# A second raw tile, loads in another order, statistics one tile per period, and another cut of the last odd fold in a three-stage kernel

## What is computed

```python
def phi(x):
    proj = einsum('bhsd,df->bhsf', x, w_phi)            # 64 -> 128
    proj = proj - max(abs(proj), axis=-1, keepdims=True)
    return concatenate([exp(proj), exp(-proj)], axis=-1)
q_p, k_p = phi(q), phi(k)
kv, z = einsum('bhsf,bhsd->bhfd', k_p, v), sum(k_p, axis=2)
x = einsum('bhsf,bhfd->bhsd', q_p, kv) / (einsum('bhsf,bhf->bhs', q_p, z) + 1e-6)
u = x + real(fft(fft(x, axis=1), axis=2))               # heads joined to 512 columns
y = u + relu(layernorm(u) @ w1a) @ w2a                  # w1: 512 x 2048, w2: 2048 x 512
out = y + relu((layernorm(y) * g) @ w1b) @ w2b
```

## Time and profile before

| | us |
|---|---|
| median of 3 runs (lowest to highest) | 1062.37 (1058.77 to 1062.54) |
| the profiled execution | 1061.2 |
| its span | 1059.1 |
| PE busy | 1043.5 |
| DVE busy | 668.2 |
| ACT busy | 527.9 |
| POOL busy | 382.2 |

### The profile page before, as it was taken

The page is one execution under the profiler, slowest core; times in us unless marked ns, Lnnn a source line. Parts: engine busy times, 40 slices in busy tenths (PEclk is TensorE's granted clock), DMA queues, the critical chain, the costliest instruction groups (busy, mean ns, idle before and its releaser), DMA issues.

```text
span 1059.1 us, 17436 instructions
## 1 busy us (share of the span) xinstructions
PE 1043.5 (99%) x6294; PEld 964.1 (91%) x6294; DVE 668.2 (63%) x1155; ACT 527.9 (50%) x958; POOL 382.2 (36%) x365
## 2 busy tenths in 40 slices
PE   8999999999899999999999999999999999999998
PEld 8999999999889899899898899889899899999897
DVE  5675776798775557754586564864568554674443
ACT  5756565676544436344354445444454444544341
POOL 4413333254343426242451433523444323532210
PEclk9999999999999999999999999999999999999999
DMA  5242121210123121222122122222114221142201
GB/s 140 69 108 68 35 69 35 67 46 13 56 65 119 50 72 60 75 65 81 42 79 78 43 80 60 64 77 69 52 61 139 61 80 60 60 135 77 61 7 60
DMA packets 68626, 72.47 MB, mean 68 GB/s; under 512 B 24256, under 2 KB 49088, under 8 KB 68544
## 3 DMA queue, kind: packets, MB, share of 16 engines
q1 hardware_dynamic: 68384, 71.30, 22.6%
q10 hardware_dynamic: 160, 0.07, 0.0%
HBM read 66.10 MB, written 4.72 MB: 67 GB/s over the span
## 4 chain that ended last, share of the span: by engine, by line
PE 88%; DVE 6%; issue 2%; ACT 2%; DMA 1%; SPq 1%; POOL 1%; DVEq 0%; ACTq 0%; POOLq 0%
PE bank L1102 34%; PE bank L1079 30%; PE bank L383 6%; PE bank L369 5%; PE bank L331 4%; PE bank L352 3%; PE bank L616 2%; PE bank L596 2%; PE bank L1038 2%; DVE stats L1384 2%; DMA rawqk<-qkT 1%; PE bank L325 1%; DVE hid L1358 1%; DVE w1op L1286 1%; DVE part_s L1328 0%
## 5 line engine op out<-in xcount | busy, mean ns | idle before, releaser
L1102 PE MATMUL bank<-w2op,hid 128*128 128x512 f32 x1728 | 426.1, 391 | 0.0
L1102 PEld LDWEIGHTS bank<-w2op,hid 128*128 128x128 f32 x1728 | 321.8, 188 | 56.6 <-issue 0.5
L1079 PE MATMUL bank<-x_T,w1op 128*128 128x384 f32 x1152 | 208.9, 336 | 0.0
L1079 PEld LDWEIGHTS bank<-x_T,w1op 128*128 128x128 f32 x1152 | 201.7, 188 | 3.8
L1250 POOL TENSOR_TENSOR w_sums<-st_w 128x256 f32<-128x256 f32 x48 | 44.8, 933 | 411.2 <-DVE w1op L1286 405.2
L1079 PE MATMUL bank<-x_B,w1op 128*128 128x384 f32 x864 | 176.2, 339 | 0.9 <-DVE part_s L1328 0.9
L1079 PEld LDWEIGHTS bank<-x_B,w1op 128*128 128x128 f32 x864 | 151.9, 188 | 10.0 <-issue 1.3
L1299 DVE TENSOR_TENSOR w2op<-st_w,w2op 128x1024 fp32r<-128x1024 f32 x48 | 65.8, 1372 | 98.7 <-ACT w2op L1295 98.7
L1358 DVE SCALAR_TENSOR_TENSOR hid<-part_s,hid 128x384 fp32r<-128x384 f32 x141 | 97.5, 718 | 37.3 <-ACT hid L1354 37.1
L1354 ACT ACTIVATE hid<-part_s 128x384 fp32r<-128x384 f32 x141 | 72.9, 524 | 28.6 <-DVE part_s L1328 28.3
L399 POOL TENSOR_TENSOR qk_lo<-rawqk,qk_hi 128x640 fp32r<-128x640 f32 x28 | 42.7, 1548 | 119.8 <-ACT qk_hi L393 119.8
(11 more groups left out here) (171 smaller groups left out, 1610.3 us busy)
## 6 DMA issues: line engine op xcount, KB each, us to landing
st_w<-w1a SPq DMA_DIRECT2D x24, 512.0 KB, 3.4
st_w<-w2a SPq DMA_DIRECT2D x24, 512.0 KB, 3.7
st_w<-w1b SPq DMA_DIRECT2D x24, 512.0 KB, 3.3
st_w<-w2b SPq DMA_DIRECT2D x24, 512.0 KB, 3.7
rawqk<-qkT SPq DMA_DIRECT2D x16, 288.0 KB, 3.8
rawqk<-qkT SPq DMA_DIRECT2D x16, 256.0 KB, 4.0
v<-v SPq DMA_DIRECT2D x16, 256.0 KB, 3.1
out<-xall SPq DMA_DIRECT2D x16, 256.0 KB, 2.1
```

Source lines behind the costliest of these rows:

```text
L1079: last = nc.tensor.matmul(dst, w1op[g % 2][:, a, W1OP.index(w), c, :], xop[x][:, b, c, :], start=name in ("M2", "M1", "M7") and k_ == 0, s ...
L1102: last = nc.tensor.matmul(acc[t0 + t][:, :], hid[name, g % 2][:, x, P * t:P * (t + 1)], w2op[g % 2][:, y, j, :], start=first and k_ == 0, ...
```

## The change

Pair 1 gets a raw tile of its own (`rawqk_second`), with its own zeroing by POOL and loading semaphore; the other pairs keep the shared tile. The two halves of w_phi are loaded first, one by SP and one by ACT; q of pair 0 comes by SP and k by ACT, with a semaphore each, and pair 1's load follows at once. The values of pair 0, pair 2's load and the constants come behind that. PE does 23 instead of 26 transposes of the identity first, the 26 in the middle go, and in slot 1 the first three units of pair 1 run before the transposes of round 0 and the 22 transposes of the identity. POOL makes the low part of pair 1. ACT and POOL split all constants in slot 2.

The two W1 loads of slot 4 are issued in slots 4 and 6. The root of the first block moves inside slot 13. The statistics get a second set of tiles, and those of block i + 2 are made one tile per period in periods 2 to 7 of block i; those of block 1 stand in the last batch's part (four tiles) and behind it (two). The root of the next block moves to period 0, the reciprocal to the head of period 1.

For the last fold the odd part no longer waits for the extra row, and the extra row waits for the odd part. POOL's even fold no longer waits for DVE's odd fold, but its next two low parts wait for the low parts of W1's second block. The orders of ACT, DVE and PE in that part change.

```diff
@@ -104,14 +104,14 @@
-    stats, o = at("stats", [P, BT, 6], F32, o)
-    mv, o = at("mv", [P, BT, 2], F32, o)
+    stats, o = at("stats", [P, 2, BT, 6], F32, o)
+    mv, o = at("mv", [P, 2, BT, 2], F32, o)
+    rstd, o = at("rstd", [P, 2, BT], F32, o)
...
-    rstd, o = at("rstd", [P, BT], F32, o)
-    wphi, o = at("wphi", [P, FEAT], F32, o)
...
-    pad, o = at("pad", [P, 1], F32, o)
...
+    wphi, o = at("wphi", [P, FEAT], F32, KEEP)
+    raw_second, o = at("rawqk_second", [P, 2, QW], F32, o)
@@ -238,10 +238,11 @@
-    s_qk, s_v, s_zero, s_w0 = sem("qk_loaded"), sem("v_loaded"), sem("zeros_ready"), sem("w_phi_split")
+    s_qk, s_v, s_zero, s_w0 = [sem("qk_even_loaded"), sem("qk_odd_loaded")], sem("v_loaded"), sem("zeros_ready"), sem("w_phi_split")
...
+    s_first, s_zero2, s_w0_lo = [sem("first_q_loaded"), sem("first_k_loaded")], sem("second_zeros_ready"), sem("w_phi_lo")
@@ -385,19 +386,27 @@
+    def raw_qk(g):
+        return raw_second if g == 1 else rawqk
+    def act_first_hi(act, w):
+        act.wait_ge(s_first[w], 48)
+        nc.scalar.copy(sqk["hi"][0][:, w, :], rawqk[:, w, :]).then_inc(qk_hi, 1)
...
-        act.wait_ge(s_qk, 48 * (g + 1))
+        act.wait_ge(s_qk[g % 2], 48 * ((g + 1) // 2))
...
-            nc.scalar.copy(sqk["hi"][g % 2][:, w, :], rawqk[:, w, :]).then_inc(qk_hi, 1)
-    def split_lo(eng, unit, g):
-        for w in range(2):
+            nc.scalar.copy(sqk["hi"][g % 2][:, w, :], raw_qk(g)[:, w, :]).then_inc(qk_hi, 1)
+    def split_lo(eng, unit, g, parts=(0, 1)):
+        for w in parts:
...
-            unit.tensor_tensor(sqk["lo"][g % 2][:, w, :], rawqk[:, w, :], f32(sqk["hi"][g % 2][:, w, :]), ALU.subtract)\
-                .then_inc(qk_lo, 1)
+            unit.tensor_tensor(sqk["lo"][g % 2][:, w, :], raw_qk(g)[:, w, :], f32(sqk["hi"][g % 2][:, w, :]),
+                               ALU.subtract).then_inc(qk_lo, 1)
@@ -498,15 +507,25 @@
+    QK_PARTS = ((slice(D, P), slice(0, MT * P), slice(0, MT * P)),
+                (slice(0, D), slice(0, S), slice(0, S)),
+                (slice(D, P), slice(MT * P + TAIL, QW), slice(MT * P, S)))
+    def load_first(eng, w):
+        for k_, (rows, dst, cols) in enumerate(QK_PARTS):
+            if k_ == 1:
+                eng.wait_ge(s_zero, 1)
+            eng.dma_start(rawqk[rows, w, dst], qkT[0][rows, w, cols]).then_inc(s_first[w], 16)
...
-        need(sp, qk_lo, 2 * g)
-        need(sp, qk_hi, 2 * g)
-        if g == 0:
-            sp.wait_ge(s_zero, 1)
-        for rows, dst, cols in ((slice(0, D), slice(0, S), slice(0, S)),
-                                (slice(D, P), slice(0, MT * P), slice(0, MT * P)),
-                                (slice(D, P), slice(MT * P + TAIL, QW), slice(MT * P, S))):
-            sp.dma_start(rawqk[rows, :, dst], qkT[g][rows, :, cols]).then_inc(s_qk, 16)
+        if g == 1:
+            sp.wait_ge(s_zero2, 1)
+        else:
+            need(sp, qk_lo, 2 * g if g > 2 else 2)
+            need(sp, qk_hi, 2 * g if g > 2 else 2)
+        for rows, dst, cols in QK_PARTS:
+            sp.dma_start(raw_qk(g)[rows, :, dst], qkT[g][rows, :, cols]).then_inc(s_qk[g % 2], 16)
@@ -619,6 +638,8 @@
+        if (b, h) == (B - 1, 1):
+            act.wait_ge(o_done, 4 * B)
@@ -644,7 +665,8 @@
-        eng.wait_ge(s_exrow, 2 * (q_ + 1))
+        eng.wait_ge(fin, H * b + 4 * (h + 1))
+        eng.wait_ge(s_exrow, 2 * (q_ + (q_ < 2 * B - 1)))
@@ -802,7 +824,13 @@
         if l >= 0 and g > 1:
             pe_transpose(pe, l, 0)
         for u in range(3):
+            if g == 0 and u == 2:
+                pe.wait_ge(s_w0, 2)
+                pe.wait_ge(s_w0_lo, 2)
             pe_unit(pe, g, u)
+        if g == 1:
+            pe_transpose(pe, l, 0)
+            pe_warm_on(pe, bank[5], WARM - 4)
         if l < 0:
             pe_unit(pe, g, 3)
             pe_unit(pe, g, 4)
@@ -934,10 +962,15 @@
+        if g == 2:
+            act.wait_ge(s_raw, 16 * 5)
+            act_const_hi(act, "cs")
...
-            for n in ("cd", "sd", "alt"):
-                act_const_hi(act, n)
+            act_const_hi(act, "ss")
+            act_const_hi(act, "cd")
+        if g == STD_SLOT:
+            act_std(act, 0)
@@ -947,13 +980,15 @@
+        if g == 2:
+            act_const_hi(act, "sd")
...
+        if g == 2:
+            act_const_hi(act, "alt")
...
-        if g == STD_SLOT:
-            act_std(act, 0)
@@ -1119,9 +1154,9 @@
         pe_product(pe, 0, "M1")
         pe_stepA(pe, B - 1, "S1")
         pe_product(pe, 0, "M6")
+        pe_product(pe, 0, "M7")
         pe_stepA(pe, B - 1, "C1")
         pe_stepA(pe, B - 1, "CX")
-        pe_product(pe, 0, "M7")
         for name in B_OUT[:HT]:
             pe_stepB(pe, B - 1, name)
         pe_product(pe, 0, "M5")
@@ -1377,31 +1412,29 @@
-            if i == NB - 1:
+            if BT * i + tiles[-1] >= len(FULL):
...
-        need(dve, mv_done, BT * i)
+        need(dve, xn_done, BT * (i - 1))
...
-            nc.vector.bn_stats(stats[:, t, :], utile(i, t)).then_inc(st_done, 1)
-        need(dve, xn_done, BT * i)
-        need(dve, sd_done, i)
+            nc.vector.bn_stats(stats[:, i % 2, t, :], utile(i, t)).then_inc(st_done, 1)
...
-            nc.vector.bn_aggr(mv[:, t, :], stats[:, t, :]).then_inc(mv_done, 1)
+            nc.vector.bn_aggr(mv[:, i % 2, t, :], stats[:, i % 2, t, :]).then_inc(mv_done, 1)
...
-        nc.scalar.activation(std[:, :], mv[:, :, 1], ACT.Sqrt, bias=epsc[:, 0:1]).then_inc(sd_done, 1)
+        nc.scalar.activation(std[:, :], mv[:, i % 2, :, 1], ACT.Sqrt, bias=epsc[:, 0:1]).then_inc(sd_done, 1)
...
-        nc.vector.reciprocal(rstd[:, :], std[:, :]).then_inc(rs_done, 1)
+        nc.vector.reciprocal(rstd[:, i % 2, :], std[:, :]).then_inc(rs_done, 1)
...
-        nc.vector.tensor_scalar(xn[k % 2][:, :], utile(i, t), mv[:, t, 0:1], rstd[:, t:t + 1],
+        nc.vector.tensor_scalar(xn[k % 2][:, :], utile(i, t), mv[:, i % 2, t, 0:1], rstd[:, i % 2, t:t + 1],
@@ -1433,8 +1466,6 @@
-            if n == 1 and nxt:
-                act_std(act, i + 1)
@@ -1443,6 +1474,8 @@
+            if n == 0 and nxt:
+                act_std(act, i + 1)
@@ -1463,8 +1496,8 @@
-                dve_ln_stats(dve, i + 1, range(BT))
-            late = n == FP_ - 1 or n == 1
+                dve_ln_rstd(dve, i + 1)
+            late = n == FP_ - 1
@@ -1477,14 +1510,14 @@
-            if n == 1 and nxt:
-                dve_ln_rstd(dve, i + 1)
...
+            if n >= TR0 and i + 2 < 2 * NB:
+                dve_ln_stats(dve, i + 2, range(n - TR0, n - TR0 + 1))
@@ -1550,19 +1583,20 @@
-            sp_qk(sp, 0)
+            sp.dma_start(wphi[0:D, :], w_phi).then_inc(s_const, 16)
+            load_first(sp, 0)
+            sp_qk(sp, 1)
...
+            sp_qk(sp, 2)
...
-            sp_qk(sp, 1)
...
-                if g + 1 < PAIRS:
+                if 1 < g < PAIRS - 1:
...
-                if g == 4:
-                    sp_w1(sp, 0)
-                    sp_w1(sp, 1)
+                if g in (4, 6):
+                    sp_w1(sp, g // 2 - 2)
@@ -1583,6 +1617,7 @@
+            nc.gpsimd.memset(raw_second[:, :, MT * P:QW], 0.0).then_inc(s_zero2, 1)
@@ -1595,13 +1630,13 @@
+                if g == 0:
+                    pool.wait_ge(qk_lo, 2)
+                    split_lo(pool, nc.gpsimd, 1)
...
-                if g == 0:
-                    for n_, n in enumerate(("cs", "ss")):
+                if g == 2:
+                    for n_, n in enumerate(("cs", "ss", "cd", "sd")):
...
-                if g == 2:
-                    for n_, n in enumerate(("cd", "sd")):
-                        split_const(pool, nc.gpsimd, 2 + n_, n)
@@ -1614,8 +1649,8 @@
-            pool.wait_ge(oo_done, 2 * B)
...
+            pool.wait_ge(w1_lo, 6)
@@ -1626,25 +1661,24 @@
-            for half in range(2):
-                act.dma_start(wphi[D * half:D * (half + 1), :], w_phi).then_inc(s_const, 16)
+            act.dma_start(wphi[D:P, :], w_phi).then_inc(s_const, 16)
+            load_first(act, 1)
...
-                nc.scalar.copy(wbd["hi"][rows, FEAT * a:FEAT * (a + 1)], wphi[rows, :])
+                last = nc.scalar.copy(wbd["hi"][rows, FEAT * a:FEAT * (a + 1)], wphi[rows, :])
+            last.then_inc(s_w0, 1)
+            act_first_hi(act, 0)
...
-            act_split_qk(act, 0)
+            act_first_hi(act, 1)
+            act_split_qk(act, 1)
...
-            act_split_qk(act, 1)
+            act_q_copy_out(act, 0, 0)
...
-            act.wait_ge(s_raw, 16 * 5)
-            act_q_copy_out(act, 0, 0)
-            act_const_hi(act, "cs")
...
-            act_const_hi(act, "ss")
+            act_split_qk(act, 2)
...
-            act_split_qk(act, 2)
@@ -1665,23 +1699,23 @@
             act_x_hi(act, 0, 2)
             act_x_hi(act, 0, 3)
+            t_split(act, B - 1, "S0", True)
             act_exrow(act, B - 1, 1)
-            t_split(act, B - 1, "S0", True)
+            act_fold_hi(act, B - 1, 1, True)
             t_split(act, B - 1, "C0", True)
```

(36 more changed lines are left out.)

## The result

The median falls from 1060.57 us (four runs, 1058.19 to 1062.54) to 1049.95 us (four runs, 1049.78 to 1050.14): a ratio of 0.9903, with a 95% interval of 0.988 to 0.9927. The forecast was 1051.1. The profiled execution took 1050.14 us with a span of 1048.2, against 1061.2 and 1059.1 before.

The account below looks back on a forecast made before the run. PE, busy in 99% of the span, was taken as the bound, so savings had to come from its time line. Gains 2.3 + 1.8 + 0.5 + 1.7 + 1.8 + 2.0 = 10.1 us took 1061.2 to 1051.1 us, range 1046.5 to 1056.0.

Parts of the forecast that it names:

- A: The start: new PE order and earlier pair 1 load gain 1.8 us, earlier first projection 0.5; 2.3 us in all.
- rival (1): At the start, the first projection doesn't move: A is 1.8 us, total 1051.6 us; chance 0.15.
- B: W1 loads: one instead of two ahead of pair 6's load lets its cast start earlier; gain 1.8 us (1.3 to 1.9).
- C: Slot 13: root and its table load move two copies ahead, exponentials of q come earlier; gain 0.5 us (0.2 to 0.7).
- D: Last batch's fold: earlier Fourier steps, no half clock, but DVE late with two collisions; gain 1.7 us (0 to 4.4).
- E: First expert block: six statistics leave its second period and PE's waits behind them go; gain 1.8 us (0.9 to 2.2).
- F: Next four expert blocks: waits before the transposes go, 0.5 us each; gain 2.0 us (1.6 to 2.4).
- (5): Slower: with fewer warm matmuls PE stays at the lower clock through slots 0 and 1, costing 19 us, 1070.1; chance 0.03.

Follow-up runs that it names:

- q_first: Changed kernel with pair 0's q spread over both queues ahead of its k: q's cast at 5.46 us instead of 6.77, first product of keys and values 0.66 us earlier.
- root_back: Changed kernel with the first block's root on ACT again directly ahead of slot 13's exponentials of q: slot 12's to slot 14's numerators 32.44 us, against 31.50.
- pool_free: Changed kernel without POOL's wait for the second W1 block's low parts: 20.37 us from the tail's first step to the first output product, instead of 22.11.
- stats_back: Changed kernel with the later blocks' six statistics again together in period 1 of the block before: 557.38 us from the 29th to the 169th output group, 2.37 more.
- before_again: The kernel before, profiled again with nothing altered: 3.9 us between the two profiles, slot 4's to slot 5's numerators 18.76 us instead of 17.08.
- order_back: Changed kernel with PE's start order as before the change, loads as changed: first numerator at 28.33 us, 3.28 later than in the changed kernel.
- w1_back: Changed kernel with both W1 loads again in slot 4: slot 4's to slot 5's numerators 15.35 us, 0.37 more, and to slot 6's 14.37, 0.57 more.
- w1_parts_back: Changed kernel with both W1 loads in slot 4 and the old order of a raw load's parts from pair 2 on: 15.12 and 14.49 us, together 0.83 more.

## Why the prediction came out as it did

The forecast was 1.1 us too high, and the range held. Its sum went by terms, and each term has its stretch of the time line. That the total came so close is in part luck: single terms missed by 0.25 to 0.81 us, upwards and downwards, and the misses leave 0.85 us. The second profile of the kernel before took 3.9 us longer than the one that the sum started from.

- **A**, 2.3 predicted (1.8 for the order, 0.5 for the first projection), 1.65 measured. The order was right: 1.60, with the predicted 0.9 us of waiting for DVE's shift_k seen as 0.79, and pair 1's cast at 9.17, within the 9.3 that it had. The 0.5 failed: w_phi was cast at 4.62 instead of 5.50, and q's cast moved by 0.05 us, so the wait for w_phi had not been the bound. This is rival (1). The Trainium skill, "DMA: Bandwidth & Descriptors", section "Issuing engines are not separate DMA queues", says that starting transfers from several engines saves only the time to issue them. q_first agrees: the split that shortens q's issues moves the cast by 1.3 us.
- **Slots 2 to 4** lost 0.33 us that no term had; it is chance, as the second profile has nothing of it.
- **B**, 1.8 predicted, 2.10 and 0.13 measured. The size is near, the reason only in part: putting both loads back costs 0.83 to 0.94 us, or less, since a second profile of the unaltered kernel had 0.37 of it too. The prediction took the whole wait of 3.16 us in the earlier trace rows for the bytes ahead. 1.2 to 1.3 us of the gain appear only where pair 6's own issue is late as well, as in both profiles of before (2.5 us instead of 0.55). The prediction didn't have this issue, so that B came out near its size is in part luck.
- **C**, 0.5 predicted, 0.95 measured, above its bound of 0.7. The mechanism was right, shown by root_back. The bound was PE's listed wait of 0.64 us; the stall that it stands for was 1.05.
- **D**, 1.7 predicted, 2.51 measured. That PE's Fourier steps would run at the full clock and nearly without wait, and that two collisions would stand in front of the last sum, was right; they cost 1.40 and 0.97 us, not 1.6 each. Two steps failed. S1 comes 0.52 us earlier than before (5.18 us behind S0 instead of 5.70), not 0.8; yet the new place of the extra row is worth 1.80, because without it the even fold, which no longer waits for the odd one, runs beside it. And the even fold's 0.56 us was put down to POOL's wait, which isn't needed for it: pool_free has it too, and the wait costs 1.74 us. The 4.4 us that the prediction gave PE alone is what pool_free has (24.62 - 20.37 = 4.25). The four statistics, which the sum put on DVE's path with 2.8 us, cost nothing.
- **E**, 1.8 predicted, 1.55 measured. A new wait was expected at W2's second load; it came at POOL's four weight sums, behind the mixes, which ACT's cast of the W1 sums waited for (idle 3.40 us until 303.49).
- **F**, 2.0 predicted, 2.39 measured, at the upper bound. stats_back shows the mechanism. Here too the listed waits, 1.6 us, stand for more.
- Of the slower rivals, (5), the clock at the start, did occur in four experiments and in before_again, but for 2 to 3 us only, and costs 0.9 to 1.6 us, not 19. It isn't a matter of the three identity products fewer: the kernel before has them.

## What to carry to other kernels

Take the price of a stall from start to start of the same instruction in two stretches that are otherwise alike; the list of waits gave 0.6 us where the time line lost 1.05, and 1.6 where it lost 2.37. A wait that keeps one engine out of another's way only moves the collision: ask what it will meet next, and who waits for that (here a fold that was safe anyway was bought with 1.74 us). Before a transfer is put on a second queue, count how many issues stand ahead of its last part on its own queue.

## What the runs showed of the hardware

- PE ran the first projections at half clock in five of fourteen profiles: four experiments whose first 8 us are those of the changed kernel, and the kernel before. In order_back the identity products ahead had never left the pace of 0.21 us. In the others they had reached 0.11, PE paused 2.2 to 2.4 us, and the granted clock read 0.50; with pauses of 0.7 to 2.1 us it read 1.00 in nine. What decides isn't settled.
- The same two 512 KB loads, issued at the same place, landed in 6.9 and 7.0 us in one kernel and in 4.3 in another with the same bytes on the queue.
- The first issue of pair 6's load took SP 2.54 and 2.45 us in the two profiles of before, with a fetch of instructions beside it, and 0.55 in w1_back and w1_parts_back without one. Over all profiles 67 of the 77 issues of over 1.0 us (between 20 and 1000 us) overlap such a fetch.
- Two-input instructions of DVE beside POOL lost 0.7 to 1.4 us each (0.56 to 1.26 and 1.39, 0.55 to 1.95, 1.22 to 2.19); the statistics lost nothing.
